# GpSimd's two additions of a step's outputs wait for VectorE's sixth pair of the next step

## The chip, the cores and the metric

The kernel runs on one core of a Trainium2 chip. The metric is the device time of one execution in microseconds. Three runs of the kernel before gave a median of 1274.24 us (1273.68 to 1275.58).

A core has five engines that matter here. TensorE (PE, with its weight loads PEld) multiplies matrices. VectorE (DVE), ScalarE (ACT) and GpSimd (POOL) work on tiles. SyncE (SP) only issues DMAs. Each engine runs its own list in order, and they wait for one another on semaphores (counters). Work tiles lie in SBUF, products of TensorE in PSUM.

## The reference

A position-dependent causal mixing over seven taps is followed by a two-layer network with a squared ReLU:

```python
w = exp(weight_gen - max) ; w = w / (sum(w) + 1e-9)          # softmax over K = 7 taps
out = np.einsum('bshk,bskhg->bshg', w, x_unf)                # B=4, S=4096, D=192, 8 heads of 24
h = x @ w_in                                                 # 16384 x 192 by 192 x 2048
r = np.maximum(h, 0.0)
g = s * (r * r) + b
return (g @ w_out).astype(np.float32)                        # 2048 x 192
```

Everything is float32.

## The kernel before, in words

**Tiling.** The 16384 tokens lie as 128 partitions by 128 tokens. A step takes four tokens of every partition, 512 tokens in all, so there are 32 steps (0 to 31). The hidden layer has 16 tiles of 128 features. They are taken in four groups of four, and each group is two pairs, so a step has eight pairs, 0 to 7.

**Numbers in two parts.** To keep float32 precision, each factor is held as a high part and a low part. For pair q of a step, ScalarE takes the ReLU (L392) and the square (L396) into `r`. The high part `g_hi` is a copy by ScalarE for even pairs (L403) and a cast by VectorE for odd pairs (L542). VectorE then subtracts to get `g_lo` (L546). Each of these subtractions adds one to the semaphore `g_lo_ready`.

**TensorE's order.** Within a step TensorE takes first product 0, then the second product of the step before's last group, then first product 1, second product 0, first product 2, second product 1, first product 3, second product 2. A first product (L671) makes `h` of a group in PSUM. A second product (L693 with `g_hi`, L701 with `g_lo`) adds a group's contribution to the outputs `op`. A second product waits for both pairs of its group: for second product 0 these are pairs 0 and 1.

**The transposes.** In the middle of second product 2 TensorE transposes the mixed inputs of the next step (L631 and L637). They read `attn_a` and `attn_b`, which VectorE writes at the end of the seven taps of that step (L518, L519). TensorE waits for them on `sum_ready`, ahead of the last `g_lo` products of the first quarter of second product 2. After the transposes ScalarE and VectorE make `xT` (L378, L381, L384, L524, L528, L532), which first product 0 of the next step needs.

**VectorE's order in step i.** It makes the low part of `xT`, the shift of the weights, pairs 6 and 7 of step i-1, the normalised weights, taps 0 to 2 of step i+1, pairs 0 and 1 of step i, tap 3, pair 2, tap 4, pair 3, tap 5, pairs 4 and 5, and then tap 6: one product (L499), one sum (L514), and the two last sums into `attn_a` and `attn_b`.

**The outputs.** A step's outputs are whole after its last second product, which runs inside the next step. ScalarE copies them out of PSUM, scaled, into `out_sums` (L411), behind the square of pair 1. GpSimd adds the two halves (L355) and the bias (L360, into `out_sb`), and SyncE stores `out_sb`. For the last step VectorE does this work itself. GpSimd has nothing else to do in the loop.

Of the kernel before, what the change touches and what calls it, by code (L numbers as in the profile page):

```python
# [37 lines left out]
def mix_and_mlp(nc, x, weight_gen, moe_w_in, moe_w_out, moe_s, moe_b, out):  # L38
# [9 lines left out]
    PAIRS = 2 * NG  # L48
# [13 lines left out]
    with ExitStack() as ctx:  # L62
# [3 lines left out]
        def sem(name):  # L66
            return ctx.enter_context(nc.semaphore(name))
# [89 lines left out]
        g_lo_ready = sem("g_lo_ready")  # L157
# [35 lines left out]
        def zero_batch_start(engine, i, q):  # L193

            first = q * (S // TOK)
            return engine.memset(x_in[first:first + 1, i, 0:PAD - STEP * i, :], 0.0)
# [79 lines left out]
        @block.gpsimd  # L276
        def _(pool):


            steps = 0  # L280

            def stepped(instruction):
                nonlocal steps
                instruction.then_inc(pool_step, 1)
                steps += 1
                pool.wait_ge(pool_step, steps)

            for i in range(2):
                stepped(nc.gpsimd.memset(x_in[0:1, i, 0:PAD - STEP * i, :], 0.0))
            stepped(nc.gpsimd.memset(ones[:, :], 1.0))  # L290
            nc.gpsimd.affine_select(out=ident[:, :], in_=ones[:, :], compare_op=ALU.is_equal, fill=0.0,
                                    base=0, pattern=[[-1, P]], channel_multiplier=1).then_inc(ident_ready, 1)
            pool.wait_ge(ident_ready, 1)

            pool.wait_ge(x_halo_loaded[0], 2 * FETCH)
            zero_batch_start(nc.gpsimd, 0, 1).then_inc(halo_zeroed, 1)

            def split_w1(g):
                cols = slice(g * GROUP * P, (g + 1) * GROUP * P)
                half_cols = slice(g * PAIR * P, (g + 1) * PAIR * P)  # L300
                pool.wait_ge(w1_loaded[g], 3 * FETCH)
                pool.wait_ge(w1_hi_ready, g + 1)
                nc.gpsimd.tensor_tensor(w1_lo[:, cols], w1_raw[:, cols], w1_hi[:, cols].bitcast(F32), ALU.subtract)
                nc.gpsimd.tensor_tensor(w2_lo[:, half_cols], w2_raw[:, half_cols], w2_hi[:, half_cols].bitcast(F32),
                                        ALU.subtract).then_inc(w1_lo_ready, 1)

            def split_wo(g):
                tiles = slice(g * GROUP, (g + 1) * GROUP)
                pool.wait_ge(wo_loaded[g], FETCH)
                pool.wait_ge(wo_hi_ready, g + 1)  # L310
                nc.gpsimd.tensor_tensor(wo[:, tiles, 1, :], wo_raw[:, tiles, :], wo[:, tiles, 0, :].bitcast(F32),
                                        ALU.subtract).then_inc(wo_lo_ready, 1)

            def taps_of_last_token():

                pool.wait_ge(w_soft_ready, 1)
                pool.wait_ge(x_loaded[0], FETCH)
                pool.wait_ge(halo_zeroed, 1)
                pool.wait_ge(dve_zeroed, B - 2)
                for k in range(K):  # L320
                    product = acc[:, DVE_TOK, :] if k == 0 else tap_pool[:, k % 2, :]
                    if k > 2:
                        pool.wait_ge(pool_sum_ready, k - 2)
                    nc.gpsimd.tensor_tensor(product.rearrange("p (h g) -> p h g", h=H),
                                            x_in[:, 0, DVE_TOK + k, :].rearrange("p (h g) -> p h g", h=H),
                                            w_soft[:, DVE_TOK, :, k].unsqueeze(2).to_broadcast([P, H, G]),
                                            ALU.mult).then_inc(pool_tap_ready, 1)
                    if k > 0:
                        pool.wait_ge(pool_tap_ready, k + 1)
                    if k > 1:  # L330
                        pool.wait_ge(pool_sum_ready, k - 1)
                    if 0 < k < K - 1:
                        nc.gpsimd.tensor_tensor(acc[:, DVE_TOK, :], acc[:, DVE_TOK, :], tap_pool[:, k % 2, :],
                                                ALU.add).then_inc(pool_sum_ready, 1)
                    if k == K - 1:
                        nc.gpsimd.tensor_tensor(attn_a[:, DVE_TOK, :], acc[:, DVE_TOK, 0:P], tap_pool[:, k % 2, 0:P], ALU.add)
                        nc.gpsimd.tensor_tensor(attn_b[:, DVE_TOK, :], acc[:, DVE_TOK, P:D], tap_pool[:, k % 2, P:D],
                                                ALU.add).then_inc(pool_sum_ready, 1)

            taps_of_last_token()  # L340
            split_w1(0)
            split_w1(1)
            split_wo(0)
            split_w1(2)
            split_wo(1)
            split_w1(3)
            split_wo(2)
            split_wo(3)

            def add_sums(i, first=False):  # L350

                if first:
                    pool.wait_ge(bias_ready, 1)
                pool.wait_ge(out_sums_ready, i + 1)
                nc.gpsimd.tensor_tensor(out_sums[:, :, 0:D], out_sums[:, :, 0:D], out_sums[:, :, D:2 * D],  # L355
                                        ALU.add).then_inc(out_added, 1)
                if not first:
                    pool.wait_ge(out_stored, FETCH * i)
                pool.wait_ge(out_added, i + 1)
                nc.gpsimd.tensor_tensor(out_sb[:, :, :], out_sums[:, :, 0:D], bias[:, :].unsqueeze(1).to_broadcast([P, STEP, D]),  # L360
                                        ALU.add).then_inc(out_ready, 1)

            add_sums(0, first=True)
            with pool.Fori(1, STEPS - 1) as i:
                add_sums(i)
# [407 lines left out]
```

## Time and profile before

| | |
|---|---|
| median of three runs | 1274.24 us |
| the profiled execution | 1271.76 us |
| its span | 1269.8 us |
| PE busy | 1175.0 us, 93% of the span |
| VectorE busy | 994.1 us, 78% |
| ScalarE busy | 783.2 us, 62% |
| GpSimd busy | 162.1 us, 13% |
| TensorE's mean granted clock | 0.98 |
| store of a step's outputs, issue to landing | 2.3 us |

The span is what the profiler sees from the first instruction to the last. The execution's own time is 2.0 us longer. Busy shares are means over the whole run; what a change is worth is read from the stretch of a step in which it acts. Times in the rows below are microseconds from the span's start.

### The profile page before, as it was taken

To read this page: it belongs to the slowest core of one execution; us is meant where nothing else is said; L and a number is where in the kernel's file an instruction comes from. 1 tells how busy PE (TensorE), PEld (TensorE's weight loads), DVE (VectorE), ACT (ScalarE), POOL (GpSimd) and SP (SyncE) were. 2 spreads that over 40 slices of the span, in tenths; PEclk is the share of its full clock that TensorE was granted. 3 is DMA by queue.
4 is the path that set the end of the run, shared out by engine and by line. 5 is a ranking of instruction groups with operands and counts; after the bars stand their busy time and mean duration, and the time that the engine had idled before them with its cause. 6 is when DMAs were issued, how large, how long until landed. Compare 5 with 4: busy or idle time off the path is not lost.

```text
span 1269.8 us, 32095 instructions
## 1 busy us (share of the span) xinstructions
PE 1175.0 (93%) x13216; PEld 1063.1 (84%) x13216; DVE 994.1 (78%) x1162; ACT 783.2 (62%) x844; POOL 162.1 (13%) x97
## 2 busy tenths in 40 slices
PE   4899999999999999999999999999999999999998
PEld 3798888888988888988889888889888888888987
DVE  7888777888777787778887788877778877888763
ACT  3476665666655666656666666676556665556764
POOL 7311101111011111011110011110111110111100
PEclk8899999999999999999999999999999999999999
DMA  6011110111110111101111101111001111011000
GB/s 180 24 49 48 35 47 12 47 47 47 35 40 19 47 47 37 45 12 47 47 47 35 47 12 47 47 47 35 31 29 47 47 35 47 12 47 47 12 1 26
DMA packets 18409, 51.06 MB, mean 40 GB/s; under 512 B 2140, under 2 KB 9691, under 8 KB 18394
## 3 DMA queue, kind: packets, MB, share of 16 engines
q1 hardware_dynamic: 18245, 50.27, 11.7%
q10 hardware_dynamic: 149, 0.59, 0.2%
q8 instruction: 10, 0.16, 0.1%
q14 instruction: 5, 0.04, 0.0%
HBM read 38.27 MB, written 12.58 MB: 40 GB/s over the span
## 4 chain that ended last, share of the span: by engine, by line
PE 53%; DVE 29%; ACT 9%; issue 7%; POOL 1%; DVEq 1%; DMA 0%; ACTq 0%; POOLq 0%
PE hp L671 22%; PE op L693 21%; DVE g_lo L546 13%; PE op L701 10%; DVE g_hi L542 7%; DVE tap L499 3%; ACT r L396 3%; ACT g_hi L403 3%; DVE acc L514 2%; ACT xT L381 2%; ACT xT L384 1%; DVE w_soft L479 1%; DVE w_rec L477 1%; DVE w_sum L473 1%; DVE acc L499 1%
## 5 line engine op out<-in xcount | busy, mean ns | idle before, releaser
L693 PE MATMUL op<-wo,g_hi 64*128 64x384 f32 x4096 | 627.2, 367 | 71.0 <-DVE g_lo L546 71.0
L701 PE MATMUL op<-wo,g_lo 64*128 64x192 f32 x4096 | 525.9, 252 | 0.0
L392 ACT ACTIVATE r<-hp 128x1024 f32<-128x1024 f32 x256 | 258.0, 1021 | 407.4 <-PE hp L671 392.3
L671 PE MATMUL hp<-xT,w_hi 64*128 64x512 f32 x3072 | 481.9, 391 | 3.1 <-ACT r L392 1.9
L546 DVE TENSOR_TENSOR g_lo<-r,g_hi 128x1024 fp32r<-128x1024 f32 x256 | 359.7, 1405 | 150.2 <-ACT g_hi L403 145.8
L693 PEld LDWEIGHTS op<-wo,g_hi 64*128 64x128 f32 x4096 | 396.2, 189 | 87.7 <-DVE g_lo L546 74.9
L701 PEld LDWEIGHTS op<-wo,g_lo 64*128 64x128 f32 x4096 | 402.6, 192 | 10.0 <-issue 4.6
L671 PEld LDWEIGHTS hp<-xT,w_hi 64*128 64x128 f32 x3072 | 281.4, 185 | 57.8 <-ACT r L392 1.8
L671 PE MATMUL hp<-xT,w_lo 64*128 64x512 f32 x1536 | 304.9, 392 | 0.0
L396 ACT ACTIVATE r<-r 128x1024 f32<-128x1024 f32 x256 | 270.9, 1058 | 6.8
L355 POOL TENSOR_TENSOR out_sums<-out_sums 128x768 f32<-128x768 f32 x31 | 62.2, 2005 | 1064.1 <-ACT out_sums L411 1064.1
L499 DVE TENSOR_TENSOR tap<-x_in,w_soft 128x768 f32<-128x768 f32 (+1 forms) x192 | 185.0, 977 | 0.1
L671 PEld LDWEIGHTS hp<-xT,w_lo 64*128 64x128 f32 x1536 | 145.9, 185 | 30.0
L542 DVE CAST g_hi<-r 128x1024 fp32r<-128x1024 f32 x128 | 134.4, 1050 | 25.9 <-ACT r L396 23.2
L514 DVE TENSOR_TENSOR acc<-acc,tap 128x768 f32<-128x768 f32 (+1 forms) x160 | 154.5, 966 | 0.0
L403 ACT ACTIVATE g_hi<-r 128x1024 fp32r<-128x1024 f32 x128 | 135.7, 1060 | 11.0
L360 POOL TENSOR_TENSOR out_sb<-out_sums,bias 128x768 f32<-128x768 f32 x31 | 65.5, 2113 | 4.4
L524 DVE TENSOR_TENSOR xT<-hp,xT 128x512 fp32r<-128x512 f32 x32 | 22.1, 692 | 44.9 <-ACT xT L378 44.9
L411 ACT ACTIVATE out_sums<-op,s_col 128x1536 f32<-128x1536 f32 x31 | 47.9, 1545 | 0.5 <-PE op L701 0.4
L528 DVE TENSOR_TENSOR xT<-hp,xT 64x256 fp32r<-64x256 f32 x64 | 27.0, 421 | 24.7 <-ACT xT L381 24.2
L381 ACT ACTIVATE xT<-hp 64x256 fp32r<-64x256 f32 x64 | 24.3, 379 | 22.2 <-PE hp L637 21.8
L499 DVE TENSOR_TENSOR acc<-x_in,w_soft 128x768 f32<-128x768 f32 (+1 forms) x32 | 32.0, 1000 | 6.5 <-DVE w_soft L479 6.3
(42 smaller groups left out, 275.1 us busy)
## 6 DMA issues: line engine op xcount, KB each, us to landing
x_in<-in_x SPq DMA_DIRECT2D x30, 960.0 KB, 4.8
out<-out_sb SPq DMA_DIRECT2D x31, 384.0 KB, 2.3
w_in<-in_weight_gen SPq DMA_DIRECT2D x32, 112.0 KB, 2.0
wo_raw<-in_moe_w_out SPq DMA_DIRECT2D x4, 384.0 KB, 7.3
w_raw<-in_moe_w_in SPq DMA_DIRECT2D x4, 256.0 KB, 5.5
x_in<-in_x SPq DMA_DIRECT2D x1, 768.0 KB, 5.8
x_in<-in_x ACTq DMA_DIRECT2D x1, 540.0 KB
w_raw<-in_moe_w_in SPq DMA_DIRECT2D x8, 64.0 KB, 4.9
```

The source lines that it names most:

```text
L355: nc.gpsimd.tensor_tensor(out_sums[:, :, 0:D], out_sums[:, :, 0:D], out_sums[:, :, D:2 * D], ALU.add).then_inc(out_added, 1)
L360: nc.gpsimd.tensor_tensor(out_sb[:, :, :], out_sums[:, :, 0:D], bias[:, :].unsqueeze(1).to_broadcast([P, STEP, D]), ALU.add).then_inc(out_ ...
L392: nc.scalar.activation(r[:, b, :], hp[:, PAIR * b:PAIR * (b + 1), :], ACT.Relu).then_inc(relu_done, 1)
L396: nc.scalar.activation(r[:, q % 2, :], r[:, q % 2, :], ACT.Square).then_inc(square_done, 1)
L403: nc.scalar.activation(g_hi[:, q // 2 % 2, 0:PAIR, :], r[:, 0, :].rearrange("p (f n) -> p f n", f=PAIR), ACT.Copy).then_inc(g_hi_even_read ...
L499: nc.vector.tensor_tensor(product.rearrange("p t (h g) -> p t h g", h=H), x_in[:, parity, k:k + n, :].rearrange("p t (h g) -> p t h g", h= ...
L514: nc.vector.tensor_tensor(acc[:, 0:n, :], acc[:, 0:n, :], tap[:, k % 2, 0:n, :], ALU.add).then_inc(sum_ready, 1)
L542: nc.vector.tensor_copy(g_hi[:, buf, tiles, :], pair).then_inc(g_hi_odd_ready, 1)
L546: nc.vector.tensor_tensor(g_lo[:, buf, tiles, :], pair, g_hi[:, buf, tiles, :].bitcast(F32), ALU.subtract).then_inc(g_lo_ready, 1)
L671: mm = nc.tensor.matmul(hp[:, j, :], w, xt, start=start, stop=stop)
L693: nc.tensor.matmul(op[:, t, 0:2 * D], g_hi[rows[h], g % 2, j, t * P:(t + 1) * P], wo[rows[h], k, :, :].rearrange("p a d -> p (a d)"), star ...
L701: mm = nc.tensor.matmul(op[:, t, 0:D], g_lo[rows[h], g % 2, j, t * P:(t + 1) * P], wo[rows[h], k, 0, :], start=False, stop=(k == FT - 1 an ...
```

## The change

One wait is added in front of GpSimd's first addition. GpSimd still waits for ScalarE's copy of step i's outputs, and now also until `g_lo_ready` has counted the pairs 0 to 5 of step i+1. The index is (i + 1) x 8 pairs of the steps up to i, and six of the step i+1.

```diff
@@ -352,6 +352,7 @@
                 if first:
                     pool.wait_ge(bias_ready, 1)
                 pool.wait_ge(out_sums_ready, i + 1)
+                pool.wait_ge(g_lo_ready, (i + 1) * PAIRS + PAIRS - 2)
                 nc.gpsimd.tensor_tensor(out_sums[:, :, 0:D], out_sums[:, :, 0:D], out_sums[:, :, D:2 * D],
                                         ALU.add).then_inc(out_added, 1)
                 if not first:
```

No instruction changes its place on its engine. What changes is the moment at which GpSimd's two additions run, and with them the store that follows them.

## Rows read from the trace of the kernel before

**Rows 1.** Waits, 120 to 1190 us: who waited for whom, us, times, longest.

```profile
PE op L693 <- DVE g_lo L546: 64.6, 28, 2.3
```

**Rows 2.** TensorE's timeline: start us, length us, instruction [idle before <- releaser].

```profile
623.91 0.44 PE L693 MATMUL op<-wo,g_hi 64*128 64x384 f32 x2 [2.31 <-DVE g_lo L546]
```

**Rows 3.** VectorE's timeline, the cast and the subtraction of pair 1.

```profile
618.75 2.35 DVE L542 CAST g_hi<-r 128x1024 fp32r<-128x1024 f32 x1
621.13 2.72 DVE L546 TENSOR_TENSOR g_lo<-r,g_hi 128x1024 fp32r<-128x1024 f32 x1
```

**Rows 4.** GpSimd's timeline: additions of several steps.

```profile
192.59 1.99 POOL L355 TENSOR_TENSOR out_sums<-out_sums 128x768 f32<-128x768 f32 x1 [33.94 <-ACT out_sums L411]
...
232.34 1.98 POOL L355 TENSOR_TENSOR out_sums<-out_sums 128x768 f32<-128x768 f32 x1 [35.53 <-ACT out_sums L411]
...
618.56 1.98 POOL L355 TENSOR_TENSOR out_sums<-out_sums 128x768 f32<-128x768 f32 x1 [33.93 <-ACT out_sums L411]
620.68 2.08 POOL L360 TENSOR_TENSOR out_sb<-out_sums,bias 128x768 f32<-128x768 f32 x1
656.71 1.99 POOL L355 TENSOR_TENSOR out_sums<-out_sums 128x768 f32<-128x768 f32 x1 [33.94 <-ACT out_sums L411]
...
1159.01 1.98 POOL L355 TENSOR_TENSOR out_sums<-out_sums 128x768 f32<-128x768 f32 x1 [33.97 <-ACT out_sums L411]
...
1198.84 2.39 POOL L355 TENSOR_TENSOR out_sums<-out_sums 128x768 f32<-128x768 f32 x1 [35.63 <-ACT out_sums L411]
...
1237.23 1.84 POOL L360 TENSOR_TENSOR out_sb<-out_sums,bias 128x768 f32<-128x768 f32 x1
```

**Rows 5.** VectorE's timeline in step 1.

```profile
80.14 0.69 DVE L542 CAST g_hi<-r 128x1024 fp32r<-128x1024 f32 x1
80.87 2.76 DVE L546 TENSOR_TENSOR g_lo<-r,g_hi 128x1024 fp32r<-128x1024 f32 x1
83.55 2.60 DVE L499 TENSOR_TENSOR tap<-x_in,w_soft 128x768 f32<-128x768 f32 x1
```

**Rows 6.** GpSimd's timeline in step 1.

```profile
80.21 2.33 POOL L355 TENSOR_TENSOR out_sums<-out_sums 128x768 f32<-128x768 f32 x1 [37.27 <-ACT out_sums L411]
82.62 2.71 POOL L360 TENSOR_TENSOR out_sb<-out_sums,bias 128x768 f32<-128x768 f32 x1
```

**Rows 7.** VectorE's timeline from pair 5 to the low part of xT.

```profile
599.58 1.22 DVE L546 TENSOR_TENSOR g_lo<-r,g_hi 128x1024 fp32r<-128x1024 f32 x1
600.72 0.95 DVE L499 TENSOR_TENSOR tap<-x_in,w_soft 128x768 f32<-128x768 f32 x1
601.59 0.95 DVE L514 TENSOR_TENSOR acc<-acc,tap 128x768 f32<-128x768 f32 x1
602.67 0.69 DVE L518 TENSOR_TENSOR attn_a<-acc,tap 128x512 f32<-128x512 f32 x1
603.28 0.42 DVE L519 TENSOR_TENSOR attn_b<-acc,tap 128x256 f32<-128x256 f32 x1
605.10 0.69 DVE L524 TENSOR_TENSOR xT<-hp,xT 128x512 fp32r<-128x512 f32 x1 [1.40 <-ACT xT L378]
```

**Rows 8.** TensorE's timeline at the first transposes.

```profile
603.83 0.19 PEld L701 LDWEIGHTS op<-wo,g_lo 64*128 64x128 f32 x2 [0.16 <-issue]
...
604.03 0.41 PE L631 MATMUL hp<-ident,attn_a 64*128 64x64 f32 x8
```

**Rows 9.** Windows: each engine's busy time (instructions), granted clock, DMA share, GB/s.

```profile
46.00:48.00 2.00, 2.00 (x14) 2.00 (x16) 2.00 (x3) 1.97 (x3) 0.00 (x0) 0.50 0.00 0
663.70:667.10 3.40, 3.40 (x30) 3.40 (x28) 3.40 (x5) 0.52 (x1) 0.00 (x0) 0.50 0.00 0
```

**Rows 10.** TensorE's timeline at the start of the run.

```profile
44.17 0.69 PE L693 MATMUL op<-wo,g_hi 64*128 64x384 f32 x2 [3.76 <-DVE g_lo L546]
```

**Rows 11.** VectorE's timeline, pair 5 of step 31 and the last output.

```profile
1251.79 1.23 DVE L546 TENSOR_TENSOR g_lo<-r,g_hi 128x1024 fp32r<-128x1024 f32 x1
...
1265.04 0.62 DVE L558 SCALAR_TENSOR_TENSOR out_sums<-op,s_col,bias 128x384 f32<-128x384 f32 x1 [3.32 <-PE op L701]
```

## The prediction

> **What bounds the kernel now.** I read the waits first. In the steady steps TensorE waits for one thing only, VectorE's `g_lo`: 28 times, 64.6 us, at most 2.3 us each [rows 1]. Busy shares (93% for PE) say the same. TensorE's own work sets the time, plus what it is made to wait. So every place where it waits, and every place where it nearly does, counts in full.
>
> TensorE's timeline shows where the wait is: second product 0, at its third tile, which needs pair 1. PE stands for 2.31 us, from 621.60 to 623.91 [rows 2]. The `g_lo` it waits for ends at 621.13 + 2.72 = 623.85 [rows 3].
>
> VectorE and GpSimd side by side show why that is late. The cast of pair 1 takes 2.35 us and the subtraction 2.72 us [rows 3]. In step 1 the same cast takes 0.69 us [rows 5], and pair 5's subtraction takes 1.22 us [rows 7]. GpSimd's additions run at just these moments, 618.56 to 620.54 and 620.68 to 622.76 [rows 4]. The pattern is strict alternation. The cast is issued at 618.75, after GpSimd began. It ends at 621.10, which is 0.56 us behind the first addition. The second addition starts beside the cast and takes 2.08 us, where an undisturbed one takes 1.84 us [rows 4]. The subtraction then ends 1.09 us behind it. Each engine waits for the whole of the other's instruction. The delay to pair 1 is (2.35 - 0.69) + (2.72 - 1.22) = 3.16 us, of which TensorE sees 2.31 us, so there were about 0.85 us of slack.
>
> **What the change takes away.** With GpSimd silent there, pair 1 is ready near 620.7 (618.75 + 0.69 + 1.22 and a few hundredths between), 0.9 us ahead of TensorE's arrival. All of 28 x 2.31 = 64.6 us goes [rows 1]. Steps 1 and 30 wait less there, and I leave them out.
>
> **What it adds.** GpSimd is released when pair 5's subtraction ends, at 599.58 + 1.22 = 600.80 in terms of rows 7. The other new wait states, `out_sums_ready` and the earlier store, are long past. Nothing is queued behind the waiting addition but the second one and, on SP, the store. The store then goes out near 605, ahead of SP's next loads, which VectorE's weight shift releases later. ScalarE's next copy into `out_sums` comes a third of a step later. I count these three at nothing; that cover is over 3 us deep.
>
> Behind pair 5 VectorE has tap 6: a product, a sum, and the sums into `attn_a` and `attn_b`, ending at 603.28 + 0.42 = 603.70 [rows 7]. Are these held up as the subtraction was? Step 1 shows it for the same kinds: the product L499 that takes 0.95 us alone [rows 7] takes 2.60 us beside GpSimd's second addition [rows 5, 6]. There, too, the order is that of issue. GpSimd's first addition was issued at 80.21 beside the cast begun at 80.14, and went ahead of the subtraction issued at 80.87. The two operations behind the cast lose (2.76 - 1.22) + (2.60 - 0.95) = 3.19 us.
>
> The new place looks like step 1. GpSimd asks at about 600.9, while the product runs (600.72 to 601.67). So I run the rows forward, with 1.7 us for an addition that holds up the other engine (from the cast's end at 621.10 to the second addition's at 622.76 it is 1.66). First addition to 603.38. The sum L514, 0.81 us after that, to 604.19. Second addition to 605.87. `attn_a` 0.55 us later, 606.42. `attn_b` to 606.76. That is 3.06 us late, a little under the 3.19 of step 1 because VectorE's own short pause between the sum and `attn_a` is covered.
>
> Who waits for `attn_a` and `attn_b`? TensorE does, for the transposes. It resumes at 603.83, behind a pause of 0.16 us, and the transposes start at 604.03 [rows 8]. `attn_b` was ready at 603.70. The slack is at most 0.13 us. So of 3.06 us, 2.93 to 3.06 us become a stall. I take 2.95. The transposes' successors (`xT`, the first product, pairs 6 and 7) start from the transposes, so they shift with them and win nothing back. Pair 5 itself hangs on TensorE's own progress through first product 2, so VectorE can't arrive earlier either. Steps 1 to 30 have both transposes and additions: 30 x 2.95 = 88.5 us. The bounds: nothing at all if these operations were not held, and 3.19 - 0 = 3.19 us a step, 95.7 us, from step 1.
>
> The Trainium skill has this in "SBUF — State Buffer", section "Who interferes with whom": VectorE and GpSimd share a pair of SBUF ports, the one that issues first keeps it for its whole instruction and the other fully blocks, and a two-input VectorE operation in SBUF is among those that contend. It adds that the order of issue decides who blocks, not the kind of operation. By that rule GpSimd, asking at 600.9, goes ahead of the sum issued at 601.59, and the stall is as above, about 1310; if instead an engine with work in hand kept the ports, the first rival below would hold, 1235. The same section says that a VectorE operation with one SBUF input is not held, so an addition that came as late as the low part of `xT` would cost nothing. The trace agrees on the order in rows 3 to 6; no row shows an addition beside `xT`.
>
> **TensorE's clock.** The additions of successive steps are 656.71 - 618.56 = 38.15 us apart. Nine times, first from 192.59 to 232.34 and last from 1159.01 to 1198.84, it is about 39.8 us [rows 4]. In such a step there is a stretch of 3.4 us at a granted clock of 0.50 (1.2 GHz instead of 2.4) soon behind the stall [rows 9], which costs 39.75 - 38.15 = 1.6 us. The 3.76 us stall at the start is also followed by 0.50 [rows 9, 10]. So 9 of 28 stalls of 2.31 us brought the low clock, and the one long stall did too. A stall of 2.95 us should bring it more often. I take 19 of 30, between one third (as now, 10) and all 30. The added cost is (19 - 9) x 1.5 = 15 us, with bounds of about 0 and 21 x 1.6 = 34 us. I use 1.5, since part of a slow stretch may lie inside a stall.
>
> **The end.** In step 31 pair 5 is done at 1251.79 + 1.23 = 1253.02, so the two additions and the store (2.3 us) end near 1259.5, ahead of the last output at 1265.04 [rows 11]. It costs nothing.
>
> **The sum.** -64.6 + 88.5 + 15 = +38.9 us on the profiled execution's 1271.76 us, 1310.7 us. The median of the three runs is 2.5 us above the profiled one. Between the two, and leaning to fewer clock falls, I say 1310.
>
> **Rivals.**
>
> *The second addition slips behind the taps.* If VectorE's back-to-back pair (product and sum) keeps GpSimd out until its pause, the first addition goes in at the pause and the second asks while `attn_a` runs; if `attn_b` also goes ahead, only one addition delays it, 1.5 us, and TensorE stands 1.4 us. Then 30 x 1.4 = 42 - 64.6 = -23, and since stalls that short show no low clock, another -14 (9 x 1.6): -37, 1235 us. For it: `attn_a` and `attn_b` overlap by 0.08 us as back-to-back work does. Against it: in rows 3 to 6 GpSimd, asking first, always goes next.
>
> *Tap 6 isn't held up.* Then only the gain is left, -64.6 - 14 = -79, 1193 us. Only the 2.60 us product of step 1 speaks against it, and that is strong.
>
> *The wait does nothing, or both halves balance.* If the stall at the transposes were 2.2 us (0.7 us more slack than I read), time stays within a few us of 1272. The 0.16 us pause in rows 8 speaks against it.
>
> *The stall moves, but the clock doesn't get worse.* Slower side, +24 us less what the clock gives: with as many falls as now 1296, with none at all 1282. It would be so if what TensorE does around the stall matters more than its length.
>
> *Every stall brings the low clock, and the stall is 3.19 us.* 95.7 - 64.6 + 34 = +65: 1337. This is the worst of the same mechanism.
>
> **How the numbers follow.** My forecast with 13 to 25 falls: 0.60. Clock no worse: 0.20. Nearly every stall low: 0.06. Second addition slips: 0.07. Tap 6 free: 0.03. Balance: 0.04. About 0.2% (2.5 us) is what a measurement of this kernel can tell from no change. Slower holds 0.60 + 0.20 + 0.06 and half of balance, 0.88; same 0.02; faster 0.10. The range takes in the clock cases and leaves out the faster ones and the worst, 0.20 in all: 1282 to 1328.
>
> **What would show it.** In the profile after: pair 1's cast back to 0.69 us and its subtraction to 1.23 us; TensorE's wait for `g_lo` in second product 0 gone; the sum L514 and `attn_a` of tap 6 at about 2.5 and 2.2 us; a new wait of about 3 us of L701 or L631 for VectorE's `attn_b`, 30 times; more stretches at clock 0.50. A step without a low clock should take 38.15 - 2.31 + 2.95 = 38.8 us. I am wrong if `attn_b` comes less than 2.3 us late, or if TensorE had slack there that the rows hide.

## The result, and the profile after

The changed kernel takes 1309.35 us (median of four runs, 1308.03 to 1309.86) against 1274.07 us for the kernel before. The ratio is 1.0273, with a 95% interval of 1.0255 to 1.0291: slower by 2.7%. The profiled execution took 1309.58 us (span 1307.6 us), 37.8 us more than the profiled one before.

**The wait moved from pair 1 to the transposes.** These are the waits of the whole changed kernel, in us, times and longest. L702 and L520 are L701 and L519 of before, one line further down.

```profile
PE op L702 <- DVE attn_b L520: 88.5, 30, 3.0
...
PE op L694 <- DVE g_lo L547: 5.1, 4, 3.4
```

The 64.6 us of [rows 1] are gone; what is left of that wait (four times, 5.1 us) is at the start and the end of the run. In their place TensorE waits 30 times for `attn_b`.

**VectorE is held at tap 6, and no longer at pair 1.** First GpSimd's, then VectorE's timeline, start and length in us, then TensorE where it resumes.

```profile
613.30 2.49 POOL L356 TENSOR_TENSOR out_sums<-out_sums 128x768 f32<-128x768 f32 x1 [33.67 <-DVE g_lo L547]
615.94 2.33 POOL L361 TENSOR_TENSOR out_sb<-out_sums,bias 128x768 f32<-128x768 f32 x1
```

```profile
612.00 1.22 DVE L547 TENSOR_TENSOR g_lo<-r,g_hi 128x1024 fp32r<-128x1024 f32 x1
613.14 0.95 DVE L500 TENSOR_TENSOR tap<-x_in,w_soft 128x768 f32<-128x768 f32 x1
614.01 2.60 DVE L515 TENSOR_TENSOR acc<-acc,tap 128x768 f32<-128x768 f32 x1
616.74 2.08 DVE L519 TENSOR_TENSOR attn_a<-acc,tap 128x512 f32<-128x512 f32 x1
618.75 0.41 DVE L520 TENSOR_TENSOR attn_b<-acc,tap 128x256 f32<-128x256 f32 x1
...
635.16 0.68 DVE L543 CAST g_hi<-r 128x1024 fp32r<-128x1024 f32 x1
635.88 1.23 DVE L547 TENSOR_TENSOR g_lo<-r,g_hi 128x1024 fp32r<-128x1024 f32 x1
```

```profile
619.29 0.36 PE L702 MATMUL op<-wo,g_lo 64*128 64x192 f32 x2 [2.95 <-DVE attn_b L520]
```

The engines take turns. `[2.95 <-DVE attn_b L520]` means that TensorE stood idle for 2.95 us before this matmul, until `attn_b` was written. GpSimd asks at 613.30, while the tap's product runs, and its first addition ends at 615.79. The sum L515, issued at 614.01, ends 0.82 us behind it. The second addition, asked for during the sum, ends at 618.27, and `attn_a` 0.55 us behind it. From pair 5's end to `attn_b`'s end it takes 619.16 - 613.22 = 5.94 us, where it took 603.70 - 600.80 = 2.90 us [rows 7]: 3.04 us late. TensorE had no slack here at all: it resumes 0.13 us behind `attn_b`'s end now (619.29), as it did before (603.83 behind 603.70). Pair 1 is back to 0.68 and 1.23 us, where [rows 3] had 2.35 and 2.72.

**The clock falls more often, and at times for twice as long.** These are GpSimd's first additions in four successive steps.

```profile
613.30 2.49 POOL L356 TENSOR_TENSOR out_sums<-out_sums 128x768 f32<-128x768 f32 x1 [33.67 <-DVE g_lo L547]
...
653.40 2.50 POOL L356 TENSOR_TENSOR out_sums<-out_sums 128x768 f32<-128x768 f32 x1 [35.13 <-DVE g_lo L547]
...
693.51 2.50 POOL L356 TENSOR_TENSOR out_sums<-out_sums 128x768 f32<-128x768 f32 x1 [35.14 <-DVE g_lo L547]
...
734.68 2.50 POOL L356 TENSOR_TENSOR out_sums<-out_sums 128x768 f32<-128x768 f32 x1 [36.19 <-DVE g_lo L547]
```

In a fall the granted clock goes from 1.00 to 0.50 for a while (2.4 GHz and 1.2 GHz). The distances here are 40.10, 40.11 and 41.17 us. Over the run 10 of 30 are 38.6 us (these steps have no fall), 16 are 40.1 and four are 41.2. The windows of the last kind (busy time by engine, then the granted clock) show why: the clock falls inside the stall, before TensorE resumes at 699.50, and stays low until after 705.

```profile
697.00:698.00 1.00, 0.00 (x0) 0.00 (x0) 1.00 (x1) 0.00 (x0) 1.00 (x1) 1.00 0.00 0
698.00:699.00 1.00, 0.00 (x0) 0.00 (x0) 1.00 (x2) 0.00 (x0) 0.48 (x1) 0.72 0.00 0
699.00:700.00 1.00, 0.49 (x6) 0.50 (x8) 0.37 (x2) 0.00 (x0) 0.00 (x0) 0.50 0.52 206
...
704.00:705.00 1.00, 1.00 (x10) 1.00 (x10) 0.95 (x3) 0.97 (x2) 0.00 (x0) 0.50 0.00 0
705.00:706.00 1.00, 1.00 (x16) 1.00 (x16) 0.79 (x3) 0.89 (x2) 0.00 (x0) 0.86 0.00 0
```

A single fall lasts 3.4 us, as in [rows 9]; this one lasts 6.8.

### The profile page after: what moved, and what is told of

The parts are those of the page before. It is cut to its first block and busy times, and to the rows that moved or that the text cites. A ratio compares the mean times of both kernels' runs of the same rounds, so it can differ in the third digit from the quotient of the medians.

```text
span 1307.6 us, 32125 instructions
## 1 busy us (share of the span) xinstructions
PE 1190.8 (91%) x13216; PEld 1091.9 (84%) x13216; DVE 993.1 (76%) x1162; ACT 778.3 (60%) x844; POOL 183.0 (14%) x97
## 5 line engine op out<-in xcount | busy, mean ns | idle before, releaser
L694 PE MATMUL op<-wo,g_hi 64*128 64x384 f32 x4096 | 639.3, 374 | 5.1 <-DVE g_lo L547 5.1
L702 PE MATMUL op<-wo,g_lo 64*128 64x192 f32 x4096 | 540.7, 256 | 88.5 <-DVE attn_b L520 88.5
L702 PEld LDWEIGHTS op<-wo,g_lo 64*128 64x128 f32 x4096 | 420.1, 197 | 100.9 <-issue 96.1
L547 DVE TENSOR_TENSOR g_lo<-r,g_hi 128x1024 fp32r<-128x1024 f32 x256 | 315.0, 1231 | 173.5 <-ACT g_hi L404 167.4
L694 PEld LDWEIGHTS op<-wo,g_hi 64*128 64x128 f32 x4096 | 413.6, 194 | 12.1 <-issue 3.8
L356 POOL TENSOR_TENSOR out_sums<-out_sums 128x768 f32<-128x768 f32 x31 | 76.7, 2474 | 1099.1 <-DVE g_lo L547 1099.1
L515 DVE TENSOR_TENSOR acc<-acc,tap 128x768 f32<-128x768 f32 (+1 forms) x160 | 204.4, 1278 | 0.0
L543 DVE CAST g_hi<-r 128x1024 fp32r<-128x1024 f32 x128 | 88.0, 688 | 26.0 <-ACT r L397 23.2
L379 ACT ACTIVATE xT<-hp 128x512 fp32r<-128x512 f32 x32 | 19.1, 597 | 110.7 <-PE hp L632 110.6
L519 DVE TENSOR_TENSOR attn_a<-acc,tap 128x512 f32<-128x512 f32 (+1 forms) x32 | 63.8, 1994 | 4.0
L529 DVE TENSOR_TENSOR xT<-hp,xT 64x256 fp32r<-64x256 f32 x64 | 27.0, 421 | 38.8 <-ACT xT L382 38.4
```

The costliest lines, as they stand in the source:

```text
L515: nc.vector.tensor_tensor(acc[:, 0:n, :], acc[:, 0:n, :], tap[:, k % 2, 0:n, :], ALU.add).then_inc(sum_ready, 1)
L543: nc.vector.tensor_copy(g_hi[:, buf, tiles, :], pair).then_inc(g_hi_odd_ready, 1)
L547: nc.vector.tensor_tensor(g_lo[:, buf, tiles, :], pair, g_hi[:, buf, tiles, :].bitcast(F32), ALU.subtract).then_inc(g_lo_ready, 1)
L694: nc.tensor.matmul(op[:, t, 0:2 * D], g_hi[rows[h], g % 2, j, t * P:(t + 1) * P], wo[rows[h], k, :, :].rearrange("p a d -> p (a d)"), star ...
L702: mm = nc.tensor.matmul(op[:, t, 0:D], g_lo[rows[h], g % 2, j, t * P:(t + 1) * P], wo[rows[h], k, 0, :], start=False, stop=(k == FT - 1 an ...
```

## The experiments

The edits are shown against the changed kernel unless another is named, and `...` marks code that is left out. The theory had three parts: GpSimd and VectorE hold each other up for whole instructions; the 3 us this costs VectorE count only where TensorE waits for what is behind them; and TensorE's clock adds to it. Times below are medians of four runs, and ratios are to the kernel before with their 95% intervals.

### The same wait at other places

**Behind pair 3.**

```diff
-                pool.wait_ge(g_lo_ready, (i + 1) * PAIRS + PAIRS - 2)
+                pool.wait_ge(g_lo_ready, (i + 1) * PAIRS + 4)
```

> The additions wait for pair 3 of the next step (the fourth) instead of pair 5. Theory (GpSimd and VectorE hold each other up for whole instructions; what counts is whether the roughly 3.1 us fall where VectorE has slack): they fall on tap 5, behind which VectorE stands idle for 2.2 to 4.5 us, and pair 4 has over 4 us until TensorE wants it. TensorE's wait for pair 1 is gone, no wait at the transposes, almost no stretch at half clock: 1271.8 - 66 - 14 = about 1192 us for the profiled run, ratio to before near 0.94. Rival A (delaying GpSimd at all is what costs, by the later store or a later buffer): 1300 or more. Rival B (the time lost is TensorE's clock from something else in the loop, and stalls only move): about 1240 to 1275.

Measured: 1189.4 us, 0.935 (0.9334 to 0.9366), 35.73 us a step and no fall of the clock in the loop.

**Behind pair 1.** The same edit with `+ 2`.

> The additions wait for pair 1 of the next step. Theory: they fall on tap 3, pair 1 itself is free of them. Pairs 2 and 3 come 3.1 us late, pair 3 just when TensorE wants it, so 1192 to 1200 us; if a little is lost, it is a wait of a few tenths for pair 2 or 3 in second product 1. Rival A: 1280 or more. Rival B: 1240 to 1275.

Measured: 1193.13 us, 0.9378 (0.9362 to 0.9393), 35.89 us a step. TensorE stands 0.22 us a step for `g_lo` in second product 1, the expected remainder.

**Behind the taps.**

```diff
-            def add_sums(i, first=False):
+            def add_sums(i, first=False, last=False):
...
-                pool.wait_ge(g_lo_ready, (i + 1) * PAIRS + PAIRS - 2)
+                if last:
+                    pool.wait_ge(g_lo_ready, (i + 1) * PAIRS + PAIRS - 2)
+                else:
+                    pool.wait_ge(sum_ready, (K - 1) * (i + 3))
...
-            with pool.Fori(1, STEPS - 1) as i:
+            with pool.Fori(1, STEPS - 2) as i:
                 add_sums(i)
+            add_sums(STEPS - 2, last=True)
```

> The additions wait until VectorE has written attn_a and attn_b (the last step keeps the wait for its pair 5). They begin some 3 us later than in the changed kernel, beside VectorE's work on xT. Theory with the order of issue, and the Trainium skill (SBUF - State Buffer, Who interferes with whom: one SBUF input is not held): L525 and L529 read PSUM and one SBUF tile and are not held, the cast L533 reads SBUF alone and could be; the additions end about 3.9 us after attn_b, at the time at which the cast starts, so it is held by a few tenths at most. No stall for attn_b: 1192 to 1205 us. Rival C (everything VectorE does beside GpSimd is held): xT comes 1.5 to 3 us late and TensorE waits for it in first product 0: 1240 to 1300 us.

Measured: 1184.95 us, 0.9315 (0.93 to 0.9331), 35.60 us a step and no fall of the clock in the loop. GpSimd's timeline, and VectorE's beside it:

```profile
634.69 1.85 POOL L359 TENSOR_TENSOR out_sums<-out_sums 128x768 f32<-128x768 f32 x1 [31.77 <-DVE attn_b L524]
636.68 1.84 POOL L364 TENSOR_TENSOR out_sb<-out_sums,bias 128x768 f32<-128x768 f32 x1
```

```profile
636.02 0.69 DVE L529 TENSOR_TENSOR xT<-hp,xT 128x512 fp32r<-128x512 f32 x1 [1.41 <-ACT xT L383]
637.49 0.86 DVE L533 TENSOR_TENSOR xT<-hp,xT 64x256 fp32r<-64x256 f32 x2 [0.78 <-ACT xT L386]
638.38 0.43 DVE L537 CAST xT<-xT 64x512 fp32r<-64x512 f32 x1
```

Both additions run at their free 1.84 us, and the first subtraction for `xT`, with one input in PSUM, keeps the 0.69 us that it had in [rows 7]. The two after it, wholly beside the second addition, take 0.42 us each, as in the kernel before. This doesn't extend to every instruction with a single input in SBUF: the cast of pair 1 has one, and it took 2.35 us beside GpSimd [rows 3]. The prediction shortens the rule of the Trainium skill, "SBUF — State Buffer", section "Who interferes with whom": it exempts an instruction with at most one SBUF input only outside VectorE's two-port modes, and it names casts among those that can enter such a mode. Three places from pair 1 to behind the taps give 1185 to 1193 us; pair 5 gives 1309. Later additions and a later store cost nothing in themselves (rival A). The 79 to 87 us gained on the kernel before are real time and don't come back elsewhere (rival B).

### One addition at each place

```diff
-                pool.wait_ge(g_lo_ready, (i + 1) * PAIRS + PAIRS - 2)
                 nc.gpsimd.tensor_tensor(out_sums[:, :, 0:D], ...
...
                 pool.wait_ge(out_added, i + 1)
+                pool.wait_ge(g_lo_ready, (i + 1) * PAIRS + PAIRS - 2)
                 nc.gpsimd.tensor_tensor(out_sb[:, :, :], ...
```

> Only the second addition waits for pair 5; the first runs where it ran before. Theory: the cast of pair 1 is held 1.66 us, which leaves a wait of about 0.8 us for pair 1; tap 6 is held by one addition, which leaves 1.3 to 1.5 us at the transposes. The waits add up to 2.1 to 2.3 us a step, as before, but in two short pieces, and if the low clock comes with long stalls alone, there is none of it: 1271.8 - 64.6 + 30 x 2.2 - 14 = about 1259 us. If the clock falls by the sum of idle time, not by single stalls, about 1270 to 1275 us. If one addition alone costs as much as two (whatever holds VectorE isn't proportional to them): 1300 us.

Measured: 1265.9 us, 0.9946 (0.993 to 0.9963). TensorE's timeline shows both halves of the old and the new wait in one step:

```profile
602.14 0.36 PE L702 MATMUL op<-wo,g_lo 64*128 64x192 f32 x2 [1.56 <-DVE attn_b L520]
...
620.72 0.44 PE L694 MATMUL op<-wo,g_hi 64*128 64x384 f32 x2 [0.81 <-DVE g_lo L547]
```

The two waits are near the expected size (0.8, and 1.3 to 1.5), and the clock doesn't fall once in the loop (38.3 us a step). The time lies between the two figures expected, 1259 and 1270 to 1275 us. The idle time of 2.37 us costs more than it shows: 38.30 - 35.60 = 2.70 us a step, where the expectation counted 2.2. So it is slower per step than before without a fall (38.15) and faster in total (by 0.5%, just clear of the noise), by the clock alone.

### Tap 6 in front of pairs 4 and 5

GpSimd's wait is the changed kernel's own.

```diff
+                if not last:
+                    taps(i + 1, parity, range(6, K), x_count, halo)
                 split_g(i, 4, first)
                 split_g(i, 5, first)
-                if not last:
-                    taps(i + 1, parity, range(6, K), x_count, halo)
```

> The changed kernel with its wait for pair 5 as it is, and tap 6 taken in front of pairs 4 and 5 in VectorE's order, where VectorE stood idle for 2.2 us. Nothing with two SBUF inputs is left behind pair 5 until the next step's pair 6, so the same wait costs nothing; attn_b is early and even the 0.16 us pause at the transposes goes: 35.45 us a step and 1180 to 1185 us. If the wait for pair 5 costs by where it puts the store or by anything but what VectorE does behind it: 1280 us or more.

Measured: 1180.08 us, 0.9264 (0.9248 to 0.9279), 35.42 us a step, the fastest version. The wait for pair 5 is not bad in itself. What VectorE has behind it makes it so.

### What GpSimd must do to hold VectorE

This kernel leaves out all but four elements of each of GpSimd's additions; memsets stand for the rest.

```diff
-                nc.gpsimd.tensor_tensor(out_sums[:, :, 0:D], ...).then_inc(out_added, 1)
+                nc.gpsimd.tensor_tensor(out_sums[:, 0, 0:4], out_sums[:, 0, 0:4], out_sums[:, 0, D:D + 4], ALU.add)
+                nc.gpsimd.memset(out_sums[:, 1:STEP, :], 0.0).then_inc(out_added, 1)
...
-                nc.gpsimd.tensor_tensor(out_sb[:, :, :], ...).then_inc(out_ready, 1)
+                nc.gpsimd.tensor_tensor(out_sb[:, 0, 0:4], out_sums[:, 0, 0:4], bias[:, 0:4], ALU.add)
+                nc.gpsimd.memset(out_sb[:, 1:STEP, :], 0.0).then_inc(out_ready, 1)
```

> The changed kernel, with GpSimd's two additions cut to a tile of 4 elements each and the rest replaced by memsets of 128x1152 and 128x576, which write SBUF and read nothing; the sums of the other elements are left out. One look. If VectorE and GpSimd meet only at a read interface (the Trainium skill, SBUF - State Buffer, Who interferes with whom: a two-input operation contends with a GpSimd instruction that reads SBUF, not with one that only writes): the sum L515 and attn_a of tap 6 keep near 0.95 and 0.69 us, a small hold of a few tenths from the 4-element additions at most, stall under 0.5 us, 1185 to 1200 us. If they meet at any access: the sum and attn_a are held by the memsets' length, about 1.2 and 0.6 us, and the time is 1230 to 1250 us.

Measured, in one look: 1185.48 us beside 1274.75 us for the kernel before. GpSimd's and VectorE's timelines in one step:

```profile
632.66 0.85 POOL L357 TENSOR_TENSOR out_sums<-out_sums 128x4 f32<-128x4 f32 x1 [32.55 <-DVE g_lo L548]
633.44 1.06 POOL L358 MEMSET out_sums<- 128x1152 f32 x1
634.64 0.55 POOL L362 TENSOR_TENSOR out_sb<-out_sums,bias 128x4 f32<-128x4 f32 x1
...
1166.87 0.20 POOL L357 TENSOR_TENSOR out_sums<-out_sums 128x4 f32<-128x4 f32 x1 [32.58 <-DVE g_lo L548]
1167.01 1.06 POOL L358 MEMSET out_sums<- 128x1152 f32 x1
```

```profile
632.49 0.95 DVE L501 TENSOR_TENSOR tap<-x_in,w_soft 128x768 f32<-128x768 f32 x1
633.36 0.95 DVE L516 TENSOR_TENSOR acc<-acc,tap 128x768 f32<-128x768 f32 x1
634.44 0.69 DVE L520 TENSOR_TENSOR attn_a<-acc,tap 128x512 f32<-128x512 f32 x1
```

The sum was issued 0.08 us ahead of the memset, so its own 0.95 us alone would prove nothing. But the two run over each other, and neither is longer: at 1167.01, with VectorE idle, the memset takes the same 1.06 us. The 4-element additions, which read SBUF, are held in the same run: 0.20 us with VectorE idle (1166.87), but 0.85 us when issued beside the tap's product, ending 0.07 us behind it. So a GpSimd instruction that only writes and a two-input sum of VectorE don't hold each other up. The Trainium skill, "SBUF — State Buffer", section "Who interferes with whom", has it so: a two-input VectorE instruction contends with a GpSimd instruction that reads SBUF, not with one that only writes it. This is a single look, and the memsets are shorter than the additions. The answer is read off the rows, not off the time.

### The clock, without GpSimd

Five kernels stall TensorE at the transposes by extra work of VectorE alone. They are built on the kernel that waits behind the taps.

```diff
+        extra = sb("extra", [P, 3, STEP * D])
...
+                    if not first:
+                        for j, c in enumerate((192, 192, 176)):
+                            nc.vector.tensor_tensor(extra[:, j, 0:STEP * c]..., acc[:, :, 0:c], tap[:, k % 2, :, 0:c], ALU.add)
                     nc.vector.tensor_tensor(attn_a[:, 0:n, :], ...
```

Each number is the width of one extra addition over four tokens. This kernel has (192, 192, 176); the others are in the table.

> Built on the kernel whose additions wait for the taps (1185.0 us, 35.60 us a step, additions undisturbed). VectorE does two extra additions of 128x768 into a spare tile in front of attn_a, 0.87 us each back to back, in steps 2 on. GpSimd plays no part in the stall. TensorE should stand 1.6 to 1.75 us at the transposes, each costing 1.74 us: 1185 + 30 x 1.74 = 1237 us. If the clock falls with the length of a stall, no step shows a fall here, as in the split kernel with its 1.6 us; if any stall at this place brings falls, up to 30 x 1.5 = 45 us more.

> As the last, with three extra additions (768, 768, 704 elements, 2.54 us in all): about the delay that the stall for pair 1 cost before (38.15 - 35.60 = 2.55 us), but at the transposes and without GpSimd. If place doesn't matter and length does: period 38.15 us without a fall, 9 to 13 falls, 1185 + 76 + 14 to 20 = 1275 to 1281 us. If the place (transposes) is what makes falls frequent: 18 to 20 falls, about 1290 us.

> As the last, with 768, 768, 768 and 384 elements, 3.04 us in all: the delay of the changed kernel, made by VectorE alone. If the changed kernel's time is only the 3.04 us stall and the clock: a step 38.64 us, 18 to 22 falls, some of them long, and 1185 + 91 + 33 = 1309 us, the changed kernel's own time. Rival (GpSimd's contention costs something beyond the delay of attn_b): clearly less than 1300 us.

The middle one missed by over 40 us, so two more lengths were run beside it.

> The series of extra additions of VectorE in front of attn_a, now 768, 768 and 352 elements, about 2.2 us in all, between the 1.74 us (1243 us, 4 falls of the clock) and the 2.54 us (1332 us, a fall of double length in nearly every step). Without falls: 1185 + 30 x 2.2 = 1251 us. If falls grow with the length of the stall alone: 5 to 15 of 1.5 us, 1258 to 1273 us. If a repeating pattern can set in here too, with a fall of 2.8 us of cost in each of some 20 steps: 1300 us and more.

> As the last, with 768, 768, 768 and 160 elements, about 2.8 us, between the 2.54 us (1332 us) and the 3.04 us (1312 us, no steady pattern). Without falls: 1185 + 30 x 2.8 = 1269 us. If falls grow with the length alone, 18 to 22 of them: 1298 to 1308 us. If the steady pattern of the 2.54 us kernel (every step 40.96 us) holds over a band of lengths that reaches here: up to 1340 us, from the step on at which it sets in.

| extra work | step without a fall | delay over 35.60 | median us | ratio | falls of 3.4 us | of 6.8 us |
|---|---|---|---|---|---|---|
| 192, 192 | 37.34 | 1.74 | 1243.05 | 0.9756 (0.9738 to 0.9775) | 4 | 0 |
| 192, 192, 88 | 37.78 | 2.18 | 1286.51 | 1.0100 (1.0076 to 1.0124) | 25 | 0 |
| 192, 192, 176 | 38.14 | 2.54 | 1332.54 | 1.0481 (1.0414 to 1.0548) | 4 | 21 |
| 192, 192, 192, 40 | 38.44 | 2.84 | 1312.18 | 1.0296 (1.0275 to 1.0318) | 10 | 11 |
| 192, 192, 192, 96 | 38.67 | 3.07 | 1311.66 | 1.0297 (1.0280 to 1.0315) | 16 | 4 |
| none, changed kernel | 38.64 | 3.04 | 1309.35 | 1.0273 (1.0255 to 1.0291) | 16 | 4 |

Falls are counted in the profiled execution of each, inside the loop; every kernel here is also at half clock for a while at the start and at the end of the run. With a fall of 3.4 us a step is 1.45 us longer, with one of 6.8 us 2.5 to 2.8 us. 1.74 us brought four falls where its length alone promised none. The two lengths added later didn't meet their expectations either: 2.18 us brought 25 falls where 5 to 15, or some 20 long ones, were expected, and 2.84 us ended between its two figures. Three things follow.

The last one reproduces the changed kernel: a step longer by 0.03 us, as many falls of each kind, a time within 2.3 us (ratios 1.0297 and 1.0273), with GpSimd's additions begun only after `attn_b`. So the additions act through the delay of `attn_b` and cost nothing beyond it that shows here.

Longer stalls don't simply bring more falls. The 2.54 us stall is the worst, although it is shorter than the changed kernel's. In the profiled execution, after the first ten steps, every step is 40.9 to 41.0 us long and contains the same fall. These are its windows in such a step: TensorE stands until 657.13, and the clock has fallen just before.

```profile
656.00:657.00 1.00, 0.00 (x0) 0.00 (x0) 0.99 (x3) 0.00 (x0) 0.00 (x0) 0.86 0.00 0
657.00:658.00 1.00, 0.87 (x12) 0.88 (x14) 0.00 (x0) 0.00 (x0) 0.93 (x1) 0.50 0.00 0
...
659.00:663.00 4.00, 4.00 (x37) 4.00 (x34) 2.04 (x5) 2.41 (x4) 1.81 (x1) 0.50 0.25 98
663.00:664.00 1.00, 1.00 (x14) 1.00 (x12) 0.45 (x2) 0.89 (x2) 0.00 (x0) 0.73 0.00 0
```

Its four runs fall into two groups, 1324 to 1326 and 1340 to 1341 us. The median of 1332.54 us lies between the groups, so no execution took that long. The profiled one is of the first group. Of the other there is no trace, but there are mean granted clocks: 0.934 and 0.936 in the faster two, 0.922 and 0.920 in the slower. By an estimate from these and the spans, the slower two were at half clock for some 39 us longer. That is about six more stretches of 6.8 us, at 2.8 us each some 16 us of time, about the gap. So they would have entered the pattern some steps sooner; this is not shown step by step.

The place of a stall counts, or the small work around it. 1.74 us at the transposes brought four falls. The split kernel's 1.56 us there brought none. The old 2.31 us idle at pair 1, worth 2.55 us, brought nine falls, and about as long a delay at the transposes brought 25. The last two have the same step length to 0.01 us (38.15 and 38.14), so there it is not the period. What exactly decides a fall stays open. It is not the stall's length and place alone, since the same stall brings a fall in one step of a kernel and none in another.

## Why the prediction was right

The prediction of 1310 us met 1309.35, and the mechanism was the one named. In points:

*What goes.* TensorE's 28 waits for pair 1 went entirely, as said. Their size was under-read: I took the idle time, 2.31 us. A step of before without a fall takes 38.15 us, and one without this stall 35.60 us, so each stall was worth 2.55 us. Over the run that is 71.4 us, not 64.6. (The 35.60 us are those of the kernel that waits behind the taps. It still has the short pause at the transposes; with tap 6 early that is gone too, 35.42 us.)

*What comes.* `attn_b` came 3.04 us late, against 3.06 worked out. TensorE's idle time was 2.95 us, 30 times, exactly the term of the sum. But its price, too, was the delay, 38.64 - 35.60 = 3.04 us: 91.2 us, not 88.5. The slack of 0.13 us that the term allowed for wasn't there. The stretches of sum and `attn_a` were 2.60 and 2.08 us for the 2.5 and 2.2 expected.

*Where the idle time is whole.* The rows of TensorE's weight loads (PEld) show what the matmul rows understate. These are first the kernel before, at the transposes and at pair 1, then the changed kernel:

```profile
603.83 0.19 PEld L701 LDWEIGHTS op<-wo,g_lo 64*128 64x128 f32 x2 [0.16 <-issue]
...
623.90 0.18 PEld L693 LDWEIGHTS op<-wo,g_hi 64*128 64x128 f32 x2 [2.54 <-DVE g_lo L546]
```

```profile
619.29 0.19 PEld L702 LDWEIGHTS op<-wo,g_lo 64*128 64x128 f32 x2 [3.20 <-issue]
```

The weight loads stand 2.54 us for the stall worth 2.55, and 3.20 - 0.16 = 3.04 us more than before at the transposes, which is the price there. Added to the 35.42 us of a step in which they don't wait, their idle times give the step's length without a fall to within 0.03 us in these two kernels, in the split one (1.81 + 1.04 us) and in all five with extra work.

*Without the clock* a step is 38.64 us long, for the 38.8 expected. The 30 steps are 1159.2 us long and were 1140.7: +18.5 us where the terms said +23.9. The two smaller stalls of steps 1 and 30, left out, are about 1.3 us of this.

*The clock.* I took 19 falls of 1.5 us for 9. There were 20 in the loop, but four were of double length, which I didn't foresee. They cost 33.4 us in place of 14.3: +19.1 where I said +15. Both errors are near 5 us and of opposite sign, so the sum, 37.6 us of the 37.8 measured, hides them; that it fits so closely is luck. The reason behind this term, that a longer stall brings more falls, is not a law: a 2.54 us stall would have brought 25 falls, most of them long. The value was a fair guess for this length and no more, and that it came within one fall is luck.

*The rivals.* GpSimd did not slip behind the taps: asking first, it went first. Tap 6 was held. The clock did get worse. The store and the end of the run cost nothing: the kernel with tap 6 early has the same wait and is the fastest. The first rival's remark that stalls of 1.4 us show no low clock had no row behind it; 1.56 us in the split kernel brought none, 1.74 us brought four.

*What I didn't see* is that the same idea works. I priced only the place that the change chose. The gain of 79 us that I wrote down for a free tap 6 is what the other places reach (1185 to 1193 us, 79 to 87 us less).

## What to carry to other kernels

When two engines hold each other up, moving the work moves the delay. Read what the held engine has behind the new place and how much slack its consumer has there. Behind pair 3 the same two additions cost next to nothing; behind pair 5 the run takes 120 us longer. Price a stall by the step's length with and without it, or by the idle time of the weight loads, not by that of the matmul. Where TensorE stalls in every step, count the falls of its clock apart, and don't assume that a stall a little shorter or longer has the same number of them.

## What the runs showed of the hardware

- A two-input GpSimd addition of 1.84 us and VectorE's two-input sums in SBUF exclude each other, in the order in which they are issued (GpSimd at 613.30, ahead of the sum at 614.01): a sum of 0.95 us became 2.60, `attn_a` of 0.69 became 2.08. A GpSimd memset and the same sum run over each other at their free 1.06 and 0.95 us, while a 4-element addition of 0.20 us, which reads SBUF, takes 0.85 beside VectorE's product.
- The idle time before the resumed matmul understates a stall: 2.31 us shown cost 2.55, 2.95 cost 3.04, and 0.81 and 1.56 in one step cost 2.70. The idle time of the weight loads shows it whole: 2.54, 3.20 less the old pause of 0.16, and 1.04 + 1.81 less the 0.16.
- In the loops of these kernels half clock (0.50, 1.2 GHz) came in stretches of 3.4 or 6.8 us. With a stall at a fixed place it settled in one kernel into a state in which every step has the long stretch: 40.96 us a step instead of 38.14, and 1324 to 1341 us at a delay of 2.54 us against 1312 us at 3.07 us.
